# Attention, expert routing and a feed-forward layer in one kernel: the first expert tile is gathered into two PSUM banks, and its loaded rows are added before the last batch's products

## The reference, cut to what matters

```python
# 1 attention: pooled (every 4 positions) plus local (|i-j| < 4), 4 batches x 8 heads x 576 x 64
out_up = np.repeat(sm_attn(q_d, k_d, v_d), 4, axis=2)
out_local = np.matmul(softmax(mask(scale * q @ k.T)), v)
x = (out_up + out_local)                  # as 2304 tokens x 512
# 2 one of 8 experts for each token (argmax of cosine logits), 512 -> 1024 -> 512
for e in range(8):
    mask = expert_idx == e
    h = np.maximum(x[mask] @ w1[e], 0.0)
    out[mask] = gate_w[mask, None] * (h @ w2[e])
# 3 feed-forward, 512 -> 2048 -> 512
h = out @ w_in
return np.maximum(0.01 * h, h) @ w_out
```

## Time and profile before

| | |
|---|---|
| median of 3 runs | 872.4 us (871.78, 872.4, 882.24) |
| profiled execution | 870.14 us, span 868.4 us from first to last instruction |
| PE busy | 855.2 us, 98% of the span |
| DVE, ACT, POOL busy | 538.4, 504.7, 204.1 us |
| granted TensorE clock | 0.998 of full speed |

### The profile page before, as it was taken

One profiled execution on the slowest core, in us unless ns is written; L12 is line 12 of the kernel. 1 busy time (PEld: TensorE's weight loads), 2 busy tenths in 40 slices (PEclk: granted clock), 3 DMA queues, 4 the chain that ended last, 5 costly groups with the idle time before them and its releaser, 6 DMA issues.

```text
span 868.4 us, 16203 instructions
## 1 busy us (share of the span) xinstructions
PE 855.2 (98%) x5875; PEld 736.4 (85%) x5879; DVE 538.4 (62%) x782; ACT 504.7 (58%) x910; POOL 204.1 (23%) x279
## 2 busy tenths in 40 slices
PE   8999999999999999999999999999999999999997
PEld 5888887788888888888888989999998998999996
DVE  7677877999999999999985543233223233223222
ACT  4778887889888889888975442222222223223222
POOL 8767864921010041520010002002002002001000
PEclk9999999999999999999999999999999999999999
DMA  8678677278477467431010002002002001000000
GB/s 246 201 225 235 208 237 256 91 263 296 169 262 273 168 188 241 114 88 51 26 51 11 0 2 73 1 1 72 0 0 72 0 0 50 22 0 25 13 0 37
DMA packets 44866, 92.66 MB, mean 107 GB/s; under 512 B 4616, under 2 KB 23928, under 8 KB 40704
## 3 DMA queue, kind: packets, MB, share of 16 engines
q1 hardware_dynamic: 34752, 43.95, 17.0%
q0 software_dynamic: 9872, 47.53, 15.6%
q10 hardware_dynamic: 176, 0.31, 0.2%
HBM read 72.97 MB, written 18.81 MB: 106 GB/s over the span
## 4 chain that ended last, share of the span: by engine, by line
PE 90%; POOL 4%; DVE 2%; issue 2%; ACT 1%; DMA 0%; SPq 0%; POOLq 0%; DVEq 0%
PE banks L1049 76%; PE banks L1111 2%; PE banks L967 1%; PE banks L1056 1%; PE banks L1030 1%; PE banks L945 1%; PE banks L856 1%; POOL pin L588 1%; PE banks L909 1%; PE banks L864 1%; PE banks L1131 1%; DVE elo L1771 1%; POOL xs L614 1%; PE banks L921 1%; PE banks L825 1%
## 5 line engine op out<-in xcount | busy, mean ns | idle before, releaser
L1771 DVE TENSOR_TENSOR elo<-wslot,ehi 128x1024 fp32r<-128x1024 f32 x196 | 237.3, 1227 | 18.8 <-ACT ehi L1361 12.8
L1361 ACT ACTIVATE ehi<-wslot 128x1024 fp32r (+1 forms) x196 | 205.8, 1059 | 18.7 <-PE banks L1049 18.1
L1865 DVE SCALAR_TENSOR_TENSOR fg<-fraw 128x384 f32<-128x384 f32 x96 | 53.6, 558 | 221.3 <-ACT fraw L1485 221.3
L1485 ACT ACTIVATE fraw<-banks 128x384 f32<-128x384 f32 x96 | 47.1, 491 | 237.8 <-PE banks L1049 237.6
L1049 PE MATMUL banks<-zhi,winhi 128*128 (+1 forms) x384 | 131.3, 342 | 0.2 <-DVE winlo L1789 0.2
L1049 PE MATMUL banks<-zhi,winlo 128*128 (+1 forms) x384 | 129.4, 337 | 0.0
L1049 PE MATMUL banks<-zlo,winhi 128*128 (+1 forms) x384 | 128.9, 336 | 0.0
L1049 PE MATMUL banks<-wouthi,flo 128*128 128x512 f32 x288 | 114.0, 396 | 0.0
L1049 PE MATMUL banks<-woutlo,fhi 128*128 128x512 f32 x288 | 113.7, 395 | 0.0
L1049 PE MATMUL banks<-wouthi,fhi 128*128 128x512 f32 x288 | 112.2, 389 | 1.1 <-DVE woutlo L1789 0.9
L806 POOL DMA_INDIRECT out_x<-o_sb,row_tok x15 | 14.6, 975 | 318.7 <-ACT o_sb L1476 315.7
(11 more groups left out here) (233 smaller groups left out, 1451.0 us busy)
## 6 DMA issues: line engine op xcount, KB each, us to landing
wslot<-in_w POOLq DMA_DIRECT2D x24, 1024.0 KB, 6.5
wslot<-in_w SPq DMA_DIRECT2D x8, 1024.0 KB, 6.2
xr<-xs SPq DMA_DIRECT2D x25, 272.0 KB, 2.9
ys<-y_sb SPq DMA_DIRECT2D x25, 256.0 KB, 3.3
qb<-in_qT SPq DMA_DIRECT2D x16, 288.0 KB, 4.0
vq<-in_vtok SPq DMA_DIRECT2D x32, 144.0 KB
kb<-in_kT SPq DMA_DIRECT2D x15, 288.0 KB, 5.0
vwin<-in_vtok SPq DMA_DIRECT2D x16, 245.0 KB
```

Source lines behind the costliest of these rows:

```text
L1361: act.activation(ehi[:, ring_at(k), :], wslot[:, chunk_cols(offs[dt], matrix, half, c)], ACT.Copy).then_inc(s_ehi, 1)
L1485: act.activation(fraw[:, f % 2, :], banks[:, f % 2, 0:TB], ACT.Copy).then_inc(s_fhev, 1)
L1771: dve.tensor_tensor(elo[:, ring_at(k), :], wslot[:, chunk_cols(offs[dt], matrix, half, c)], ehi[:, ring_at(k), :].bitcast(F32), ALU.subtra ...
L1865: dve.scalar_tensor_tensor(out=fg[:, f % 2, :], in0=fraw[:, f % 2, :], scalar=0.01, in1=fraw[:, f % 2, :], op0=ALU.mult, op1=ALU.max).then ...
```

## The change

The first tile's four column groups of 128 are laid into two banks: groups 0 and 1 in bank 0, groups 2 and 3 in bank 4 (`XFIRST = (0, 4)`). The four products that add the loaded rows, with the wait for the load, move ahead of the last batch's products, to where `warm(3, 3)` was, which is removed. The last batch's products are made for both halves for its tiles 0 and 1, then for tiles 2 to 4 of the first half, then for tiles 2 to 4 of the second. Each half has a semaphore, `s_mx0` and `s_mx`. ACT rounds a half when it is there, and DVE subtracts half by half.

```diff
+        XFIRST = (0, 4)
@@ gather_rows
-                    pe.matmul(banks[:, XB, c * P:(c + 1) * P], x_sb[:, (TILES[b][0] + j) % SLOTX, c, 0:P],
-                              hot[:, at, :], start=(first and c == 0), stop=False)
+                    m = pe.matmul(banks[:, XFIRST[c // CH], c * P:(c + 1) * P], x_sb[:, (TILES[b][0] + j) % SLOTX, c, 0:P],
+                                  hot[:, at, :], start=(first and c % CH == 0), stop=(b == B - 1 and j == MT - 1 and c % CH == CH - 1))
+                return m
@@ after gather_rows(B - 2, 3, MT + 3, False, range(1, KC))
-            warm(3, 3)
+            pe.wait_ge(s_xl[0], 16)
+            for c in range(KC):
+                pe.matmul(banks[:, XFIRST[c // CH], c * P:(c + 1) * P], xr[:, 0, c * XC:c * XC + P], ident[:],
+                          start=False, stop=False)
@@ gather_x
                 pe.wait_ge(s_xr, 2 * NPAIR)
-                for j in range(MT):
-                    if j in (0, 2):
-                        pe.wait_ge(s_hot, 2 if j == 0 else 3)
+                pe.wait_ge(s_hot, 2)
+                for j in range(2):
                     gather_rows(B - 1, j, j, False)
-                pe.wait_ge(s_xl[0], 16)
-                for c in range(KC):
-                    m = pe.matmul(banks[:, XB, c * P:(c + 1) * P], xr[:, 0, c * XC:c * XC + P], ident[:],
-                                  start=False, stop=(c == KC - 1))
-                m.then_inc(s_mx, 1)
+                pe.wait_ge(s_hot, 3)
+                for half, s_half in enumerate((s_mx0, s_mx)):
+                    for j in range(2, MT):
+                        m = gather_rows(B - 1, j, j, False, range(half * CH, (half + 1) * CH))
+                    m.then_inc(s_half, 1)
@@ round_x_first (ACT)
+                act.wait_ge(s_mx0, 1)
+                act.activation(xThi[:, 0:CH * P], banks[:, XFIRST[0], 0:CH * P], ACT.Copy).then_inc(s_x0hi, 1)
                 act.wait_ge(s_mx, 1)
-                act.activation(xThi[:, 0:CH * P], banks[:, 0, 0:CH * P], ACT.Copy).then_inc(s_x0hi, 1)
-                act.activation(xThi[:, CH * P:], banks[:, 0, CH * P:], ACT.Copy).then_inc(s_x0hi, 1)
+                act.activation(xThi[:, CH * P:], banks[:, XFIRST[1], CH * P:], ACT.Copy).then_inc(s_x0hi, 1)
@@ the first tile's rest (DVE)
+            dve.wait_ge(s_x0hi, 1)
+            dve.tensor_tensor(xTlo[:, 0:CH * P], banks[:, XFIRST[0], 0:CH * P], xThi[:, 0:CH * P].bitcast(F32), ALU.subtract)
             dve.wait_ge(s_x0hi, 2)
-            dve.tensor_tensor(xTlo[:], banks[:, 0, :], xThi[:].bitcast(F32), ALU.subtract).then_inc(s_mxlo, 1)
+            dve.tensor_tensor(xTlo[:, CH * P:], banks[:, XFIRST[1], CH * P:], xThi[:, CH * P:].bitcast(F32), ALU.subtract)\
+                .then_inc(s_mxlo, 1)
```

More of the change, by code:

```diff
@@ L320, in build @@
         s_mx = sem("s_mx")
+        s_mx0 = sem("s_mx0")
         s_mxhi = sem("s_mxhi")
```

## The result

The changed kernel takes **875.61 us** (median of 21 runs, 871.52 to 884.61), the kernel before, on the same chip, 871.77 us (median of 21, 871.34 to 882.24). The medians differ by 3.8 us; the ratio of the runs is 1.0029, 95% interval 1.0017 to 1.0041. So the change costs 0.2 to 0.4%: the interval excludes no change, and the cost is far inside 2%. The time lies in the range on record, 1.5 us above the forecast of 874.1. That forecast was a difference of 1.7 us on a base of 872.4, and the base measured now is 0.6 lower: as a difference the change costs 3.8 us, more than twice the 1.7 forecast.

What follows compares the result with a forecast made beforehand. PE, busy for 98% of the span, was taken as the bound. A 2.9 us pause for the load, less 0.59 us of empty products and 0.55 us of ACT waiting, gave +1.7 on 872.4: 874.1 us, range 870.6 to 877.2.

Steps and rivals of the forecast that it cites:

- the pause alone: Main forecast at the first tile's seam: PE waits for the load at full clock, +1.7 us net of the halves; 58%.
- rival C: PE's pause before the loaded rows' products drops TensorE to half clock: 2.0 us more, +3.7 in all, 876.1 us; 14%.
- steps 2 and 3: Last batch's seam: PE pauses 2.9 us for the load, resumes at 137.05, then its 24 matmuls take 5.50 us.
- the very transfer: The profiled load of `xr`, issued at 132.75 and landing 4.2 us later, at 136.95; used to time PE's wait.
- the sister loads: The 24 other loads of the same size: fastest 2.5 us to landing, median 2.9; bounds 0.0 to +5.8 us.
- step 4: Two halves at the first tile: ACT's first rounding runs beside PE's last products, so 0.55 us of waiting goes.
- step 6: From the second stage to the end: no wait takes up the delay, so the whole +1.7 us reaches the end.
- rival B: The second stage starts later, but its loads follow the scatters' clock and absorb the delay: 872.4 us; 12%.
- a pause of 1.00 us: PE's idle time at 16.35 to 17.35 us; the next eight transposes took 1.07 us, against 1.04 after others.
- the opening products: At the kernel's start, after 1.56 us without work, ten 128x512 products took 4.30 us, at 1.2 GHz.
- Rival A: The load lands before 134.13, so no pause at the seam and the halves' gain shows: -1.2, 871.2 us; 10%.

Runs made afterwards that it cites:

- again: The changed kernel, unchanged, run again beside the kernel before: 875.03 us, +4.2, ratio 1.0046.
- fill12: The changed kernel with twelve empty products ahead of the wait for the load: four executions at 872.71 to 874.9 us; ratio over all six 1.0051.
- late: The changed kernel with the loaded rows added last in each half and the three empty products kept: 869.75 us, 1.1 below the kernel before, ratio 0.9996.
- early: The changed kernel with its load waiting for no scatter and reading another input's rows: 870.59 against 871.9 us for the kernel before, ratio 0.9998.
- moveonly: The kernel before with only the loaded rows' products and wait moved ahead, replacing the empty products; one bank, one subtraction: 875.17 us, +4.3, ratio 1.0045.
- again2: The changed kernel, unchanged, once more on another chip: five executions at 873.94 to 876.98 us against 870.92 for the kernel before.
- fill12b: The changed kernel with twelve empty products ahead of the wait, repeated on another chip: 873.37 to 874.47 us, 2.5 to 3.6 above the kernel before.

## Why the prediction held, and where it was short

The parts that were worked out from rows held; the time came out in the range for another reason. The forecast was the pause alone, +1.7 us, and what happened in most executions is rival C, pause and half clock, +3.7 by the prediction's own sum and +3.8 measured. The result is in the range because the range was drawn to take C in, and it looks nearer to the forecast than it is because the base was 0.6 us too high. That much is luck.

*The place and the pause (steps 2 and 3): right.* I had PE resuming at 137.05, which is 3.89 us after the last rank product, and the 48 records in 5.50; again resumed after 4.02 and fill12 took 5.38, so a seam of 9.39 forecast and 9.40 from these two. So close a match is partly chance: the three profiles of the changed kernel resume after 3.69, 4.02 and 5.11 us, with pauses of 2.72, 3.06 and 4.15 where 2.9 was forecast. The load's landing was well taken from the very transfer, where the median of the sister loads would have said much less.

*The halves (step 4): right, a little low.* 0.55 us was the forecast, the wait for ACT alone. Both pairs of seams give 0.81. Before, the last `ident,xr` record starts at 139.98 (139.20 + 1.06, less its own 0.275 us) and the tile's first product 0.84 us later; in late it starts at 140.33 and the first product 0.03 us later. Of the 0.84 us the timeline counts 0.56 as waiting for ACT, and the halves hide the rest as well. I take it to be the last matmul's own way through; no run measures it alone.

*The delay is passed on (step 6): right, and rival B falls.* In the chain of work of **again**, ACT's rounding of the second tile starts at 154.77, 9.18 us after the tile's first product at 145.59; before it is 150.00 - 140.82 = 9.18:

```profile
154.77 0.06 ACT xThi L1377
```

The span is 873.3 against 868.4, 4.9 us longer, and the first product 4.77 us later. After the seam PE's longest wait is again the 0.9 us for `woutlo`.

*The clock (rival C): the step that failed.* I gave the pause alone 58% and the half clock 14%. All three profiles of the changed kernel show the half clock, and 17 of its 20 runs in the first set (without the one at 884.61) are more than 2 us above the kernel before, where the pause alone would be near 1.8. The mean clock of these 17 is 0.994 to 0.998, of the other three 0.999 or 1.0. The argument against C was that a pause of 1.00 us had left no trace; that row bounds a pause a third as long, and said nothing of this one. It should have been read as no evidence, with C at least even. The price was well sized: 2.0 us from the opening products, 1.6 to 2.8 measured. The sum by C was 876.1, half a us above the result; that half is the base, since as a difference it is 3.7 against 3.8. The three executions that kept the clock (871.52, 872.3 and 872.53 us) lie 0.3 us below to 0.8 above the kernel before, which is less than the pause alone would cost; none of them was profiled, so whether the load landed sooner in them stays open.

*Rival A (the load in time):* it was not what happened, but early shows that its mechanism is right: with the load's landing moved forward the changed kernel is 1.3 us below the kernel before. That this is near A's -1.2 is chance, because A's sum has no pause and early still has one of 0.82 us; its seam is only 0.49 us shorter.

## What to carry to other kernels

A wait moved ahead of work that doesn't need it costs, on an engine that runs its instructions in order, all of its length that the engine would not have waited anyway, however short the work behind it (in moveonly a pause of 3.13 us made the seam 2.62 us longer); put the operand that arrives last into the sum last. On TensorE the pause can have a second price, since the products behind it ran at half clock in three of four profiles, for 1.6 to 2.8 us more; a kernel whose time comes in two groups is a reason to look at the granted clock right behind its longest pause. And two parts of a change should be timed apart: here the halves gain about 1 us (0.81 by the seams, 1.1 and 1.5 by the medians), and the move loses about 4.

## What the runs showed of the hardware

The half clock after a pause isn't decided by the pause's length alone: a pause of 2.72 us brought it, one of 3.13 didn't, one of 4.15 did but for a shorter time. In **again** the clock fell while PE was still waiting, in **again2** only after it had resumed. What decides it, no run here shows.

Issued between 129.7 and 132.8 us, the load landed at nearly the same time. SP issued it when the scatters of the first two batches had landed, and the time to landing made up for the difference:

```profile
129.73 0.33 SPq L493 DMA_DIRECT2D xr<-xs  x1
```

```profile
DMA to landing us min/median/max: 7.3/7.3/7.3
```

is **late**, landing at 137.0, and

```profile
131.06 0.33 SPq L493 DMA_DIRECT2D xr<-xs  x1
```

```profile
DMA to landing us min/median/max: 6.5/6.5/6.5
```

is **again**, at 137.5; the kernel before had 132.75 and 4.2, at 136.95. Issued later it did land later: at 138.5 from 133.85 in **fill12b**, at 140.4 from 136.14 in **again2**. The scatters of the batch before the last are under way all that time; that the load of 272 KB gets through only when they thin out is my reading, and no run took them away. In **early**, issued 5.5 us ahead of the last rank product (138.40 against 143.90), it took 7.25 us and still landed about 2 us sooner, against that product, than in the kernel before.
